# Attention and two feed-forward layers on one core: a second layer put into the next slot, rest tiles' products taken in turn, and a one-row product put last

## The chip, the core and the metric
The kernel runs on one core of one Trainium2 chip. A core has TensorE (matrix products, PE in the profile; its weight loads are shown apart as PEld), VectorE (DVE), ScalarE (ACT), GpSimd (POOL) and SyncE (SP, which here only issues transfers). The engines run side by side and wait for each other through semaphores. The metric is the device time of one execution in microseconds (us), lower is better. Before the change the median of three runs is 1379.33 us (1378.09 to 1381.95).

## The reference
Three stages follow one another, for 4 batches of 576 tokens, 8 heads of 64 and a model width of 512:

```
scores = q @ k.T / 8
kth    = the 32nd largest of each row of scores
attn   = softmax of the scores that are >= kth, 0 elsewhere
x      = attn @ v                                   # heads joined to (4, 576, 512)

u  = x + real(fft over tokens of fft over width of x)
un = (u - mean) / sqrt(var + 1e-6)
y  = u + relu(un @ w_ch1) @ w_ch2                   # 512 -> 2048 -> 512

xn  = (y - mean) / sqrt(var + 1e-6) * g_ln
out = y + relu(xn @ w_ch1') @ w_ch2'                # own weights
```

## The kernel before
The program is written by hand, engine by engine. Each engine walks through numbered slots s; what stands in a slot is fixed in the code, and semaphores make an engine wait where another one is late. One attention tile of up to 128 score rows by 576 belongs to each of the slots 0 to 143 (36 for a batch); after slot 143 only feed-forward work and the last batch's transform are left.

*The attention tile.* VectorE finds the 32 largest of a row in four rounds (MAX8 and MATCH_REPLACE8, function `pair`, two tiles at a time) and then multiplies the exponentials by the mask (L1122). ScalarE makes the exponentials (`exps`, L902), copies scores out of PSUM (`scores_out`, L868) and, for the second half of the tiles, reads scores that were made early and put aside in memory (`scores_in`, L891, a transfer). TensorE turns a masked tile in five transposes (`probs_T`, L667), ScalarE copies the result (`probs_out`, L909), and TensorE multiplies it by v (`values`). For two heads of 64 columns each these products write 64 PSUM partitions each, taken in turn (L690). The last 64 rows of 576 make a rest tile: its two heads stand in one tile, rows 0 to 63 and 64 to 127. There are four rest tiles in a batch, in the slots 8, 9, 26 and 27 of its 36, 16 in all. Their products are at L684: first all five chunks of one head, then all five of the other, the last chunk with 64 rows instead of 128.

*The feed-forward layers.* The work is cut into 224 units (`NUNITS`): one unit is a group of two or three token chunks by 128 of the 2048 hidden columns. `mlp1(n)` (L719) is the unit's first layer, 12 products; ScalarE's `relu_out(n)` (L962, L963) writes the hidden values, GpSimd's `unit(n)` (L500) their low part; `mlp2(n)` (L736) is the second layer, 6 or 9 products. Most slots hold one unit: in slot s TensorE does `mlp1` of that slot's unit and, after `values(s)`, `mlp2` of the last unit of slot s - 1 (`closing_at`). Twelve slots (`DOUBLE`: 52, 66, 86, 90, 96, 101, 105, 111, 121, 126, 132, 138) hold two units, n - 1 and n. The second one comes at the slot's end, after `values_back`: `mlp1(n)`, then `mlp2(n - 1)`. On ScalarE `relu_out(n)` and `highs(n)` (rounding the next units' weights, L977, L982) stand at the slot's end too.

*The transform.* The Fourier transforms are products with cosine and sine tables. A batch has ten pieces (`dft_piece(b, i)`): four over tokens, six over width (i = 4 to 9, `wid`, L775). The pieces 4, 6 and 8 add a product with one row (`alt`, L779) in the midst of an accumulation. For batches 1 and 2 a piece is made in two halves (`sides`), two pieces in each of the slots 78 to 82 and 116 to 120; batch 0's are done together in slot 37 (`SEAM`), batch 3's after the attention.

VectorE can be at most four tiles ahead of TensorE (`RING`), and TensorE can't turn a tile before VectorE has masked it. SyncE issues the weights' transfers in order; each waits for the product that last used its buffer (L444, L455, L460).

Of the kernel before, what the change touches and what calls it, by code (L numbers as in the profile page):

```python
# [8 lines left out]
P = 128  # L9
CF = S // P  # L10
TAIL = S - CF * P
C = CF + 1
# [67 lines left out]
def units_at(s):  # L80

    return [n for n in range(NUNITS) if slot_of(n) == s]
# [20 lines left out]
def second_at(s):  # L103

    return units_at(s)[1:] if s in DOUBLE else []
# [30 lines left out]
def width(c):  # L136

    return P if c < CF else TAIL
# [69 lines left out]
def build(nc, q, k, v, g2, w_raw, seq_t, wid_t, alt_t, w_low, sc_ahead, out):  # L208
# [4 lines left out]
    with ctx:  # L213
        def sb(name, shape, dt=f32):
            return ctx.enter_context(nc.sbuf_tensor(name, shape, dt))
# [13 lines left out]
        alt = sb("alt", [1, EO])  # L229
        gb = sb("gb", [P, DM])  # L230
        vn = sb("vn", [P, 2, C, 2, D + 1])
# [8 lines left out]
        pT = sb("pT", [P, 2, C * P])  # L240
# [7 lines left out]
        aT = sb("aT", [P, 4, SO])  # L248
# [23 lines left out]
        PV = Tp[:, C * P:C * P + D + 1]  # L272
# [332 lines left out]
        def _(pe):  # L605
            def scores(s):
                b, i = divmod(s, NT)
                hp, c, head = tile_of(i)
                par = hp % 2
                if i == first_tile(hp):  # L610
                    pe.wait_ge(s_qk[par], 2 * 16 * ((NHP // 2) * b + hp // 2 + 1))
                if s >= 2:
                    pe.wait_ge(s_sc_sb, s - 1 if s < RING else s)
                if c == CF:
                    for half in range(2):
                        n = slice(half * HALF, (half + 1) * HALF)
                        for h in range(2):
                            o, hd = slice(h * TAIL, (h + 1) * TAIL), slice(h * D, (h + 1) * D)
                            last = nc.tensor.matmul(Sp[o, half, 0:HALF], qT[hd, par, CF * P:S], kT[hd, par, n],
                                                    start=True, stop=True)  # L620
                else:
                    n = slice(head * HALF, (head + 1) * HALF)
                    for h in range(2):
                        hd = slice(h * D, (h + 1) * D)
                        last = nc.tensor.matmul(score_banks(s)[:, h, 0:HALF], qT[hd, par, c * P:(c + 1) * P], kT[hd, par, n],  # L625
                                                start=True, stop=True)
                last.then_inc(s_sc_ps, 1)
# [42 lines left out]
            def values(s):  # L670
                b, i = divmod(s, NT)
                hp, t, head = tile_of(i)
                par = hp % 2
                if head == 0:
                    return
                if i <= first_tile(hp) + 1:
                    pe.wait_ge(s_v[par], 3 * 16 * ((NHP // 2) * b + hp // 2 + 1))
                pe.wait_ge(s_pT_sb, s + 1)
                if t == CF:
                    for h in range(2):  # L680
                        o = slice(h * TAIL, (h + 1) * TAIL)
                        for c in range(C):
                            w = width(c)
                            last = nc.tensor.matmul(PV[o, :], pT[0:w, i % 2, c * P + o.start:c * P + o.stop],  # L684
                                                    vn[0:w, par, c, h, :], start=(c == 0), stop=(c == C - 1))
                    last.then_inc(s_pv_ps, 1)
                    return
                for c in range(C):
                    for h in range(2):
                        last = nc.tensor.matmul(OT[h * D:(h + 1) * D, :], vn[:, par, c, h, 0:D], pT[:, h, c * P:(c + 1) * P],  # L690
                                                start=(c == 0), stop=(c == C - 1))
                last.then_inc(s_pv_ps, 2)
# [50 lines left out]
            def dft_piece(b, i):  # L743
                if i == 0:
                    pe.wait_ge(s_fold, b + 1)
                    if b in (1, 2):
                        pe.wait_ge(s_rem, b)
                if b == 0:
                    if i == 0:
                        pe.wait_ge(s_ah_sb, AHEAD)  # L750
                    if i >= 4:
                        pe.wait_ge(s_pc_sb, max(4, i - 3))
                else:
                    pe.wait_ge(s_pc_sb, PIECES * b + i)
                    if b < B - 1:
                        pe.wait_ge(s_sc_sb, min(piece_slot(b, i) + RING + 1, KEPT))
                where, (sides, n) = piece(b, i), piece_cols(b, i)
                for side in range(sides):
                    o, col = where[:, side, :], slice(side * n, (side + 1) * n)
                    if i < 4:  # L760
                        for kc in range(J):
                            r = slice(0, P) if kc < HP else rest(b)
                            last = nc.tensor.matmul(o, xf[r, kc, i // 2, (i % 2) * P:(i % 2 + 1) * P], seq[r, i // 2, kc, col],  # L763
                                                    start=(kc == 0), stop=(kc == J - 1))
                            if i == 2 and kc == 0:

                                for km in range(J):
                                    r = slice(0, P) if km < HP else rest(b)
                                    mid = xs[:, 0, km, FOLD:FOLD + 1] if km < HP else U[r, chunk(b, CF), FOLD:FOLD + 1]
                                    nc.tensor.matmul(o[0:1, :], mid, seq[r, 0, km, col], start=False, stop=False)  # L770
                    else:
                        j, part = divmod(i - 4, 2)
                        to = slice(j * P, j * P + (P if j < HP else TAIL))
                        for kk in range(2):
                            last = nc.tensor.matmul(o, aT[:, 2 * part + kk, to], wid[:, part, kk, col],  # L775
                                                    start=(kk == 0), stop=(kk == 1))
                            if part == 0 and kk == 0:

                                nc.tensor.matmul(o, aT[0:1, 2, to], alt[0:1, col], start=False, stop=False)  # L779
                last.then_inc(s_pc_ps, 1)  # L780

            def un_T(t):
# [26 lines left out]
            for s in range(SLOTS):  # L809
                pieces = [(b, i) for b in range(B) for i in range(PIECES) if piece_slot(b, i) == s]  # L810
                units = units_at(s)
                if s < TILES:
                    if turns_at(s - 1):
                        pe.wait_ge(s_unT_sb, last_turn(s))
                    probs_T(s)
                    if s + RING < KEPT and s not in SCORED.values():
                        if last_piece(s) > last_piece(s - 1) > 0 or last_piece(s) == PIECES and s == SEAM + 1:
                            pe.wait_ge(s_pc_sb, last_piece(s))
                        scores(s + RING)
                if s == START[0]:  # L820
                    for t in turns_at(s):
                        un_T(t)
                if s != START[0]:
                    for n in units:
                        if n not in second_at(s):
                            mlp1(n)
                    for t in turns_at(s):
                        un_T(t)
                if s != SEAM and pieces:
                    dft_piece(*pieces[0])  # L830
                if s < TILES:
                    values(s)
                for n in closing_at(s):
                    mlp2(n)
                if s != SEAM and pieces:
                    dft_piece(*pieces[1])
                if s < TILES:
                    values_back(s)
                for n in second_at(s):
                    mlp1(n)  # L840
                    mlp2(n - 1)
                if 0 < s <= AHEAD:
                    scores_ahead(s - 1)
                if s == SEAM:
                    pe.wait_ge(s_tab, 48)
                    for b, i in pieces:
                        dft_piece(b, i)
                if s == START[0]:
                    for n in units:
                        mlp1(n)  # L850
                        if n > 0:
                            mlp2(n - 1)
                        if n in SCORED:
                            scores(SCORED[n] + RING)
# [504 lines left out]
```

## Time and profile before
| | |
|---|---|
| median of 3 runs | 1379.33 us |
| the profiled execution | 1380.66 us, of which span 1378.9 us |
| TensorE busy | 1271.3 us, 92% of the span |
| VectorE busy | 1113.0 us, 81% |
| ScalarE busy | 789.3 us, 57% |
| GpSimd busy | 348.8 us, 25% |
| granted TensorE clock, mean | 0.971 of full speed |

The span runs from the first to the last instruction; the profiled execution's own time is 1.8 us more. A busy TensorE is not one at its peak: its products are pipelined, so a row's duration is longer than the step from one start to the next, and what a group costs is read from its start to the start of what follows. Times in the rows are counted from the span's start.

### The profile page before, as it was taken

The numbers are of one execution on the slowest core, as the hardware profiler recorded it, in microseconds if no ns is written. First come the engines' busy times: TensorE is split into PE (matmuls) and PEld (weight loads), VectorE is DVE, ScalarE is ACT, GpSimd is POOL, SyncE is SP. The second block draws the span as 40 slices with busy tenths as digits, with TensorE's granted clock in tenths as the row PEclk, the third lists the DMA queues.
The fourth block names the chain that finished last, engine by engine and source line by source line (L and its number), as shares of the span: only waits on it lengthen the run. The fifth ranks groups of instructions, "written<-read, shape, count | busy, mean of one in ns | idle before, by whom it ended". The sixth has DMA issues, their size and how long they took to land.

```text
span 1378.9 us, 22760 instructions
## 1 busy us (share of the span) xinstructions
PE 1271.3 (92%) x7944; PEld 1037.2 (75%) x7944; DVE 1113.0 (81%) x2224; ACT 789.3 (57%) x1564; POOL 348.8 (25%) x308
## 2 busy tenths in 40 slices
PE   5877778999999699799998999999999999999999
PEld 2444444777777578688887788888689999999998
DVE  7999999999999988999889789975485555555553
ACT  4777765677777456575665556654344434444442
POOL 3444430122122341132233222322121121212110
PEclk8998989999999999999999999999999999999999
DMA  7899993566757656787786467663244343333342
GB/s 258 310 339 340 328 340 129 186 218 207 245 180 257 191 187 216 247 272 237 231 281 225 155 230 243 218 229 131 76 165 143 121 156 120 130 123 123 122 146 84
DMA packets 117396, 280.63 MB, mean 204 GB/s; under 512 B 29730, under 2 KB 29731, under 8 KB 117283
## 3 DMA queue, kind: packets, MB, share of 16 engines
q1 hardware_dynamic: 105522, 231.98, 51.0%
q10 hardware_dynamic: 10368, 42.47, 8.1%
q0 software_dynamic: 1392, 4.73, 1.0%
q8 instruction: 65, 1.06, 0.3%
q14 instruction: 49, 0.39, 0.1%
HBM read 235.87 MB, written 42.73 MB: 202 GB/s over the span
## 4 chain that ended last, share of the span: by engine, by line
PE 62%; DVE 30%; issue 4%; POOL 1%; ACT 1%; DMA 1%; SPq 0%; DVEq 0%; ACTq 0%; POOLq 0%
PE Big L736 24%; PE Big L719 17%; DVE top L1109 13%; DVE wk L1115 12%; PE Sp L719 7%; PE Tp L667 3%; DVE ex L1122 3%; PE Tp L690 2%; PE Sp L763 2%; PE Tp L684 1%; PE Sp L775 1%; DVE st L1201 1%; PE Tp L794 1%; PE Sp L625 1%; PE Big L763 1%
## 5 line engine op out<-in xcount | busy, mean ns | idle before, releaser
L736 PE MATMUL Big<-wr,hh 128*128 128x512 f32 x1152 | 362.6, 396 | 0.0
L719 PE MATMUL Big<-uh,wr 128*128 128x256 f32 (+1 forms) x1384 | 317.2, 319 | 7.4 <-ACT hh L963 7.4
L1109 DVE MAX8 top<-wk 128x8 f32<-128x576 f32 x432 | 304.4, 746 | 0.0
L719 PEld LDWEIGHTS Big<-uh,wr 128*128 128x128 f32 x1384 | 233.0, 191 | 26.8 <-issue 18.7
L736 PEld LDWEIGHTS Big<-wr,hh 128*128 128x128 f32 x1152 | 217.9, 189 | 41.7
L736 PE MATMUL Big<-wr,hl 128*128 128x512 f32 x576 | 238.3, 414 | 3.6 <-DVE wr L1254 2.6
L500 POOL TENSOR_TENSOR hl<-hf,hh 128x256 fp32r<-128x256 f32 (+1 forms) x123 | 105.3, 856 | 471.7 <-ACT hh L963 471.6
L719 PE MATMUL Big<-ul,wr 128*128 128x256 f32 (+1 forms) x692 | 215.5, 311 | 0.0
L1115 DVE MATCH_REPLACE8 wk<-top,wk 128x576 f32<-128x576 f32 x288 | 211.5, 741 | 0.0
L667 PE MATMUL Tp<-ident,ex 128*128 128x128 f32 x720 | 120.8, 295 | 50.5 <-DVE ex L1122 46.7
L909 ACT ACTIVATE pT<-Tp 128x640 f32<-128x640 f32 x144 | 101.4, 704 | 112.3 <-PE Tp L667 112.0
L667 PEld LDWEIGHTS Tp<-ident,ex 128*128 128x128 f32 x720 | 89.7, 150 | 94.1 <-issue 60.7
L963 ACT ACTIVATE hh<-Big 128x256 fp32r<-128x256 f32 (+1 forms) x173 | 74.6, 431 | 119.1 <-PE Big L719 119.1
L1122 DVE SCALAR_TENSOR_TENSOR ex<-sc,top,ex 128x576 f32<-128x576 f32 x144 | 119.7, 869 | 25.6 <-ACT ex L902 25.6
L719 PEld LDWEIGHTS Big<-ul,wr 128*128 128x128 f32 x692 | 132.5, 192 | 0.0
L736 PEld LDWEIGHTS Big<-wr,hl 128*128 128x128 f32 x576 | 108.8, 189 | 31.1 <-issue 10.8
L1109 DVE MAX8 top<-sc 128x8 f32<-128x576 f32 x144 | 101.6, 747 | 20.5 <-DMA sc<-sc_ahead 13.5
L1115 DVE MATCH_REPLACE8 wk<-top,sc 128x576 f32<-128x576 f32 x144 | 105.7, 741 | 0.0
L902 ACT ACTIVATE ex<-sc,nmx 128x576 f32<-128x576 f32 x144 | 103.9, 769 | 2.3
L494 POOL TENSOR_TENSOR wr<-wf,wr 128x1024 fp32r<-128x1024 f32 x32 | 75.3, 2369 | 111.3 <-DVE top L1109 110.6
L719 PE MATMUL Sp<-uh,wr 128*128 128x384 f32 (+1 forms) x408 | 99.9, 329 | 0.0
L962 ACT ACTIVATE hf<-Big 128x256 f32<-128x256 f32 (+1 forms) x123 | 50.8, 413 | 74.2 <-PE Big L719 74.2
(133 smaller groups left out, 1859.3 us busy)
## 6 DMA issues: line engine op xcount, KB each, us to landing
wf<-in_weights SPq DMA_DIRECT2D x206, 512.0 KB, 3.6
wr<-w_low SPq DMA_DIRECT2D x246, 256.0 KB, 4.3
sc<-in_weights SPq DMA_DIRECT2D x50, 512.0 KB, 3.3
sc<-sc_ahead ACTq DMA_DIRECT2D x36, 576.0 KB, 5.5
w_low<-wr SPq DMA_DIRECT2D x32, 512.0 KB, 6.5
sc_ahead<-U ACTq DMA_DIRECT2D x18, 576.0 KB, 4.7
sc_ahead<-un ACTq DMA_DIRECT2D x9, 576.0 KB, 4.0
sc_ahead<-yb ACTq DMA_DIRECT2D x9, 576.0 KB, 6.3
```

The costliest lines, as they stand in the source:

```text
L494: pool.tensor_tensor(wr[:, r, :, 1, :], wf[:, j % WFS, :, :], wr[:, r, :, 0, :].bitcast(f32), ALU.subtract).then_inc(s_wlow, 1)
L500: pool.tensor_tensor(hl[:, n % 2, 0:w], hf[:, n % 2, 0:w], hh[:, n % 2, 0:w].bitcast(f32), ALU.subtract).then_inc(s_hl[0], 1)
L667: last = nc.tensor.transpose(Tp[:, c * P:(c + 1) * P], ex[:, s % RING, c * P:(c + 1) * P], ident[:, :])
L719: last = nc.tensor.matmul(hidden(n), a[:, kd * P:(kd + 1) * P], x[:, kd, 0:P * SIZE[p]], start=(kd == 0 and j == 0), stop=(kd == KD - 1 an ...
L736: last = nc.tensor.matmul(Ac[:, j, :], a[:, n % 2, j * P:(j + 1) * P], w, start=(f == 0 and m == 0), stop=(f == KF - 1 and m == 2))
L902: nc.scalar.activation(ex[:, s % RING, 0:S], sc[:, s % RING, :], ACT.Exp, bias=nmx[:, s % RING:s % RING + 1], scale=1.0 / np.sqrt(D)).then ...
L909: nc.scalar.activation(pT[:, s % 2, :], Tp[:, 0:C * P], ACT.Copy).then_inc(s_pT_sb, 1)
L962: nc.scalar.activation(hf[:, n % 2, 0:w], hidden(n), ACT.Relu)
L963: nc.scalar.activation(hh[:, n % 2, 0:w], hidden(n), ACT.Relu).then_inc(s_h_sb, 1)
L1109: nc.vector.max(top[:, s % RING, r, :], src).then_inc(s_top, 1)
L1115: nc.vector.match_replace(out=wk[:, a, :], in_to_replace=top[:, s % RING, r, :], in_values=src, imm_value=STRUCK).then_inc(s_struck, 1)
L1122: nc.vector.scalar_tensor_tensor(out=ex[:, s % RING, 0:S], in0=sc[:, s % RING, :], scalar=top[:, s % RING, ROUNDS - 1, 7:8], in1=ex[:, s % ...
```

## The change
Three edits, all on TensorE.

1. The second layer of a double slot's first unit, `mlp2(n - 1)`, moves from the end of slot s, behind `mlp1(n)`, to slot s + 1: behind that slot's transposes and scores, in front of its `mlp1`.
2. The rest tile's products go chunk by chunk with the two heads in turn, all of them over 128 rows (the added rows of the last chunk are zeros on one side).
3. In the width pieces of the transform the one-row product comes after all products of the piece, for both halves together, and ends the accumulation.

```diff
@@ values(s), rest tile
-                    for h in range(2):
-                        o = slice(h * TAIL, (h + 1) * TAIL)
-                        for c in range(C):
-                            w = width(c)
-                            last = nc.tensor.matmul(PV[o, :], pT[0:w, i % 2, c * P + o.start:c * P + o.stop],
-                                                    vn[0:w, par, c, h, :], start=(c == 0), stop=(c == C - 1))
+                    for c in range(C):
+                        for h in range(2):
+                            o = slice(h * TAIL, (h + 1) * TAIL)
+                            last = nc.tensor.matmul(PV[o, :], pT[:, i % 2, c * P + o.start:c * P + o.stop],
+                                                    vn[:, par, c, h, :], start=(c == 0), stop=(c == C - 1))
@@ dft_piece(b, i), i >= 4
                             last = nc.tensor.matmul(o, aT[:, 2 * part + kk, to], wid[:, part, kk, col],
-                                                    start=(kk == 0), stop=(kk == 1))
-                            if part == 0 and kk == 0:
-
-                                nc.tensor.matmul(o, aT[0:1, 2, to], alt[0:1, col], start=False, stop=False)
+                                                    start=(kk == 0), stop=(kk == 1 and part == 1))
+                if i >= 4 and (i - 4) % 2 == 0:
+                    for side in range(sides):
+                        col = slice(side * n, (side + 1) * n)
+                        last = nc.tensor.matmul(where[:, side, :], aT[0:1, 2, to], alt[0:1, col], start=False, stop=True)
@@ the loop over slots, after probs_T(s) and scores(s + RING)
+                for n in second_at(s - 1):
+                    mlp2(n - 1)
@@ at the slot's end
                 for n in second_at(s):
                     mlp1(n)
-                    mlp2(n - 1)
```

TensorE's order before, from the end of slot 105's `mlp1(n)` into slot 106 (L719 is `mlp1`, L736 `mlp2`, L667 the transposes of slot 106):

```order
L719 MATMUL Big<-uh,wr 128x384 x2
L719 MATMUL Big<-ul,wr 128x384
L736 MATMUL Big<-wr,hl 128x512
L736 MATMUL Big<-wr,hh 128x512 x2
L736 MATMUL Big<-wr,hl 128x512
L736 MATMUL Big<-wr,hh 128x512 x2
L736 MATMUL Big<-wr,hl 128x512
L736 MATMUL Big<-wr,hh 128x512 x2
L667 MATMUL Tp<-ident,ex 128x128 x5
L719 MATMUL Big<-uh,wr 128x256 x2
```

The same place now (L718 is `mlp1`, L735 `mlp2`):

```order
L718 MATMUL Big<-uh,wr 128x384 x2
L718 MATMUL Big<-ul,wr 128x384
L667 MATMUL Tp<-ident,ex 128x128 x5
L735 MATMUL Big<-wr,hl 128x512
L735 MATMUL Big<-wr,hh 128x512 x2
L735 MATMUL Big<-wr,hl 128x512
L735 MATMUL Big<-wr,hh 128x512 x2
L735 MATMUL Big<-wr,hl 128x512
L735 MATMUL Big<-wr,hh 128x512 x2
L718 MATMUL Big<-uh,wr 128x256 x2
```

The nine products of the second layer have changed places with the five transposes; nothing else moved, and the rows of the other four engines are in the same order as before.

TensorE before, in slot 80, from a width piece of the transform (L775, L779) to the rest tile (L684) and the closing second layer:

```order
L775 MATMUL Sp<-wid,aT 128x129
L779 MATMUL Sp<-alt,aT 128x129
L775 MATMUL Sp<-wid,aT 128x129 x2
L779 MATMUL Sp<-alt,aT 128x129
L775 MATMUL Sp<-wid,aT 128x129
L684 MATMUL Tp<-vn,pT 64x65 x10
L736 MATMUL Big<-wr,hl 128x512
```

The same place now:

```order
L774 MATMUL Sp<-wid,aT 128x129 x4
L779 MATMUL Sp<-alt,aT 128x129 x2
L683 MATMUL Tp<-vn,pT 64x65 x10
L735 MATMUL Big<-wr,hl 128x512
```

The products are as many as before; the one-row products now stand behind one another. The ten of the rest tile stand in one row in both, since the rows don't tell the heads apart.

## Rows read from the trace of the kernel before

**Rows 1.** The page: busy tenths in 40 slices, and the chain's shares by engine

```profile
DVE  7999999999999988999889789975485555555553
...
PE 62%; DVE 30%; issue 4%; POOL 1%; ACT 1%; DMA 1%; SPq 0%; DVEq 0%; ACTq 0%; POOLq 0%
```

**Rows 2.** Busy time by stretch: us, each engine busy (count), clock, DMA

```profile
0.00:218.00 218.00, 156.51 (x1084) 95.42 (x1084) 210.92 (x451) 151.13 (x237) 79.26 (x44) 0.90 0.87 308
...
825.00:1379.00 554.00, 546.56 (x2961) 480.51 (x2959) 339.34 (x581) 254.07 (x501) 108.26 (x92) 1.00 0.44 146
```

**Rows 3.** Timeline, VectorE: start us, us, operation [idle before <-releaser]

```profile
347.29 1.42 DVE L1109 MAX8 top<-sc 128x8 f32<-128x576 f32 x2 [0.48 <-ACT sc L868]
...
534.81 0.82 DVE L1122 SCALAR_TENSOR_TENSOR ex<-sc,top,ex 128x576 f32<-128x576 f32 x1 [4.62 <-ACT ex L902]
...
695.60 1.42 DVE L1109 MAX8 top<-sc 128x8 f32<-128x576 f32 x2 [3.22 <-DMA sc<-sc_ahead]
...
808.27 0.82 DVE L1122 SCALAR_TENSOR_TENSOR ex<-sc,top,ex 128x576 f32<-128x576 f32 x1 [6.02 <-ACT ex L902]
```

**Rows 4.** Timeline, TensorE, the transposes of slots 90 and 126

```profile
581.42 1.30 PE L667 MATMUL Tp<-ident,ex 128*128 128x128 f32 x5 [5.41 <-DVE ex L1122]
...
824.73 0.74 PE L667 MATMUL Tp<-ident,ex 128*128 128x128 f32 x5 [1.17 <-DVE ex L1122]
```

**Rows 5.** Timeline, weight loads of slot 98's rest tile, first of each stretch

```profile
635.26 0.13 PEld L684 LDWEIGHTS Tp<-vn,pT 128*64 128x64 f32 x1 [0.25 <-issue]
...
635.87 0.13 PEld L684 LDWEIGHTS Tp<-vn,pT 64*64 64x64 f32 x1
...
636.13 0.13 PEld L684 LDWEIGHTS Tp<-vn,pT 128*64 128x64 f32 x1
...
636.74 0.13 PEld L684 LDWEIGHTS Tp<-vn,pT 64*64 64x64 f32 x1
...
636.99 0.19 PEld L736 LDWEIGHTS Big<-wr,hl 128*128 128x128 f32 x1
```

**Rows 6.** Timeline, a tile of whole rows in slot 97: products, first four loads

```profile
628.76 1.31 PE L690 MATMUL Tp<-pT,vn 128*64 128x128 f32 x20
...
628.76 0.20 PEld L690 LDWEIGHTS Tp<-pT,vn 128*64 128x64 f32 x4 [0.25 <-issue]
```

**Rows 7.** Timeline, TensorE, width piece of slot 81 and what follows

```profile
526.10 0.38 PE L775 MATMUL Sp<-wid,aT 128*128 128x129 f32 x2
526.41 0.48 PE L779 MATMUL Sp<-alt,aT 1*128 1x129 f32 x2
526.83 0.71 PE L775 MATMUL Sp<-wid,aT 128*128 128x129 f32 x4
527.47 0.48 PE L779 MATMUL Sp<-alt,aT 1*128 1x129 f32 x2
527.89 0.49 PE L775 MATMUL Sp<-wid,aT 128*128 128x129 f32 x2
528.30 0.27 PE L684 MATMUL Tp<-vn,pT 128*64 128x65 f32 x1
```

**Rows 8.** Timeline, TensorE and ScalarE, from slot 105 into slot 106

```profile
686.33 0.39 PE L736 MATMUL Big<-wr,hl 128*128 128x512 f32 x1
...
688.42 0.71 PE L667 MATMUL Tp<-ident,ex 128*128 128x128 f32 x5
...
689.17 0.71 ACT L909 ACTIVATE pT<-Tp 128x640 f32<-128x640 f32 x1 [0.73 <-PE Tp L667]
689.18 0.33 ACTq L891 DMA_DIRECT2D sc<-sc_ahead  x1
```

**Rows 9.** Timeline, VectorE and TensorE, slot 111 into slot 112

```profile
718.56 0.99 DVE L1122 SCALAR_TENSOR_TENSOR ex<-sc,top,ex 128x576 f32<-128x576 f32 x1
...
720.06 0.40 PE L736 MATMUL Big<-wr,hl 128*128 128x512 f32 x1
...
721.45 0.71 PE L667 MATMUL Tp<-ident,ex 128*128 128x128 f32 x5
```

## The prediction, as it was put on record before the change was run

> **What bounds the kernel now.** I read the page first. Its busy digits show VectorE at nine tenths or more in nearly all of the first 17 slices and falling later, and its chain has 62% on TensorE and 30% on VectorE [rows 1]. So there is no single bound; the two take turns. The busy times by stretch then show the ends of the picture: to 218 us VectorE works 210.9 of 218 us, so nothing that TensorE saves there can count, and from 825 us on TensorE works 546.6 of 554 us at the full clock, so everything counts [rows 2]. Between them I looked for the places where one engine hands the bound to the other, which are the waits of VectorE and of TensorE's transposes. VectorE waits at 347.29 for scores that ScalarE copies out (0.48 us), at 534.81 for slot 82's exponentials (4.62), at 695.60 for a transfer of early scores (3.22) and at 808.27 for exponentials (6.02) [rows 3]; each of these was issued behind a `probs_out` that waited for TensorE, so up to there TensorE set the pace. In the other direction the transposes wait for VectorE's mask at 581.42 (slot 90, 5.41 us) and at 824.73 (slot 126, 1.17) [rows 4].
>
> That gives this alternation: VectorE up to about 482 us (with one link to TensorE at 347); TensorE to 534.8; VectorE to 581.4; TensorE from slot 90 through slot 106 (688.4) and over the transfer to 695.6; VectorE to slot 116 (about 746); TensorE to 808.3; VectorE to 824.7; TensorE to the end. A saving on TensorE counts only inside its own stretches. It is passed on at a handover as long as the engine that receives it had waited for longer, which the waits of 4.62, 3.22 and 6.02 us allow.
>
> **Edit 2, the rest tile.** Before, the 20 records (two for each of ten products) took from 635.26 to 636.99, 1.73 us [rows 5]. The row starts split that into stretches: 8 records with 128 rows 0.61 us, 2 with 64 rows 0.26, 8 again 0.61, 2 again 0.25. The shape changes between the stretches vanish (three of them), since all products now have 128 rows and 64 columns. That alone gives one stretch of 20 at one record a time: 0.25 + 18 x 0.06 = 1.33 us, 0.40 saved.
>
> The tile of whole rows has the same two-heads-in-turn order. Its 20 records, with 128 moving columns instead of 65, take 1.31 us by the row's duration, while one after another at 0.06 x 128/65 = 0.118 each they would take 2.4 [rows 6]. So products on the two column halves do run side by side. Its first four weight loads are done within 0.20 us though a single one takes 0.13 [rows 5, 6], so the loads overlap as well. With both overlapping, the rest tile costs 0.25 + 8 x 0.06 + 0.02, about 0.75 us, and saves 1.0. The bounds are 0.40 and 1.1; I take 1.0, since rows 6 are the same instruction form but for the moving columns.
>
> The Trainium skill (TensorEngine Tiling (Array Packing), Key Properties) says that changing the tiling mode drains the engine and that different tiles load and multiply in parallel; rows 5 and 7 show the drain as some 0.14 to 0.2 us a change. It also has a rule against this edit: TensorE: Matmul & The Clock Gate, Part 3, has weight loads overlap running products only when the row group differs. Here both heads use all rows, so by it nothing would be gained beyond the changes of shape (the second rival); rows 6 speak against it.
>
> Of the 16 rest tiles those of slots 8, 9, 26, 27 lie under VectorE's work before 218 us, and 62, 63 in its stretch up to 482: nothing. 44 and 45 make the scores for 347.29 come about 2 us earlier, but VectorE waits only 0.48 there, so they give 0.48. In TensorE's stretches lie 80, 81 (before 534.8), 98, 99 (before 688.4), 116, 117 (before 808.3) and 134, 135 (at the end): eight tiles, 8.0 us.
>
> **Edit 3, the one-row product.** In slot 81 the piece has five stretches: 0.31, 0.42, 0.64, 0.42 and 0.41 us [rows 7]. Two more records in a stretch cost 0.64 - 0.41 = 0.23. Now there are eight `wid` records (0.31 + 3 x 0.23 = 1.00) and four one-row ones (0.42 + 0.23 = 0.65): 1.65 against 2.20, 0.55 saved, since two of four changes of shape are gone. That holds where the next product has another shape anyway (a rest tile or `values` behind it: slots 80, 81, 119). In 118 and 120 the second layer follows, which now pays for the refill, some 0.1 (0.41 - 0.31 of rows 7), and starts less early: 0.35 each. In slot 82 it lies behind the handover. Sum 3 x 0.55 + 2 x 0.35 = 2.35 us. With one side (batches 0 and 3) two changes stay two; only the refill moves to the next product: 0, bounds -0.1 and +0.1 for each of six.
>
> **Edit 1, the moved second layer.** TensorE's work is the same, so in a stretch that TensorE bounds it is worth nothing by itself. What it changes is that slot s + 1's transposes come one `mlp2` earlier, 2.09 us for a group of three chunks (686.33 to 688.42) and 1.39 for two (720.06 to 721.45) [rows 8, 9]. ScalarE can't use all of it: in front of `probs_out` it still has `relu_out(n)` and `highs(n)`. At slot 106 its idle time before `probs_out` is 0.73 us [rows 8], and that is the gain of the copy, of the exponentials behind it and of the transfer issued at 689.18. This transfer releases VectorE at 695.60, a handover, so 0.73 us count. Ends: 0 if the transfer's 6.4 us grow by as much; 2.1 if it also lands sooner because it now goes ahead of the weight transfer that `mlp2` releases. I take 0.73. At slot 53 the gain falls under the same 0.48 as above. At the ten other double slots no handover hangs on `probs_out(s + 1)`: 0.
>
> The price could be a new wait: behind the transposes now queue `mlp2(n - 1)`, `mlp1(n + 1)` and all that follows. The tightest place that I found is slot 112: its mask ends at 718.56 + 0.99 = 719.55, and the transposes would start at 720.06, when the second layer starts now [rows 9]. So 0.5 us are left there, and it lies in a stretch that VectorE bounds until 746: nothing. Ahead of `mlp1(n + 1)` stand the same products as before, so the wait for `relu_out(n)` has the same cover. SyncE's transfer for the buffer that `mlp2(n - 1)` frees goes out later by the five transposes, 0.5 to 0.7 us, for a unit three further on: hidden.
>
> **The sum.** 0.48 + 8.0 + 2.35 + 0.73 = 11.6 us. The profiled execution would go from 1380.66 to 1369.1; it lies 1.33 us above the median, and I take the difference from the median: 1379.33 - 11.6 = 1367.7 us.
>
> **The clock.** After the wait of 5.41 us the five transposes of slot 90 take 1.30 us, against 0.71 elsewhere [rows 4, 9]: the lower level of 1.2 GHz instead of 2.4. Slot 90 starts a TensorE stretch, so how long the lower level lasts there counts. The change shifts that moment by some us; I allow 2 us either way.
>
> **The rivals.**
> *Side by side in products only.* The weight loads go one after another; the tile costs 1.33 us, eight tiles give 3.2, the sum is 6.8 and the time 1372.5. For it: 64-column loads follow at 0.06 us in rows 5, and twice that also fits the pace of rows 6. Against it: four loads in 0.20 us. 15%.
> *The gains don't pass the handovers.* The stretches end on something that I read as TensorE's but that VectorE or the transfers set; then only the two tiles after 825 us and part of the rest count, 2 to 4 us, about 1376.5. Against it: the waits of VectorE are long. 10%.
> *A new wait in front of the transposes.* Because TensorE gets faster and reaches the transposes 1.4 to 2.1 us earlier, VectorE's mask comes too late in the double slots, and `mlp2(n - 1)`, which used to fill that time, is queued behind. It decides from the point where the mask ends after the start of the moved `mlp2`; slot 112 is 0.5 us short of it [rows 9]. The price is up to 2.1 us a slot, and clock on top: with all twelve it would be some 20 us against a gain of 11.6, so about 1386, and slower than before needs at least six of them in TensorE's own stretches. 4%.
> *The forecast.* 66%, its own range 1365.0 to 1370.5. The remaining 5% are a larger gain (the transfer sooner, a shorter time at the low clock): about 1363.
>
> **Range and chances.** From the larger gains to the side-by-side rival and its spread: 1363.5 to 1374.0. A measurement here tells about 0.3%, 4.1 us, from no change. Faster by more than that holds the forecast, the first rival, the larger gain and a little of the second: 0.87. Within it: 0.09. Slower: 0.04.
>
> **What would show it.** The rest tile's 20 records at about 0.75 us to the next start, with no 64-row form left; 1.33 means the first rival. The two-sided `alt` records as four in a row in a piece of about 1.65 us. In slots 53, 67, 87 and so on the transposes before the second layer. VectorE's wait at 347 gone, `probs_out(106)` without an idle time before it. Slot 90 starting some 3.6 us earlier, slot 116 some 6.3, slot 126 some 9.6. The prediction is wrong if TensorE's waits for the mask grow in TensorE's own stretches, or if these slots start earlier by much less than that.

## The result, and the profile after

The changed kernel takes 1363.94 us (median of four, 1362.52 to 1364.60), the kernel before 1380.64 us beside it: a ratio of 0.9879, 95% interval 0.9867 to 0.9892, or 16.7 us less. Forecast were 11.6 us less. The profiled executions are 1364.6 and 1380.66 us, their spans 1362.8 and 1378.9, 16.1 us apart. The rows below are held against these two spans, slot by slot. A slot starts where its transposes (L667) start.

From the page after, the lines that answer to [rows 1]:

```profile
DVE  7999999899999997999899889976585454646453
...
PE 57%; DVE 35%; issue 5%; POOL 1%; ACT 1%; DMA 1%; SPq 0%; DVEq 0%; ACTq 0%; POOLq 0%
```

The picture is the same, with a little of the chain gone from TensorE to VectorE. The timeline after, VectorE, at the four places of [rows 3] (start us, us, operation, [idle before <- releaser]):

```profile
345.19 0.77 DVE L1110 MAX8 top<-sc 128x8 f32<-128x576 f32 x1
...
529.27 0.82 DVE L1123 SCALAR_TENSOR_TENSOR ex<-sc,top,ex 128x576 f32<-128x576 f32 x1 [1.50 <-ACT ex L903]
...
684.12 0.76 DVE L1110 MAX8 top<-sc 128x8 f32<-128x576 f32 x1
...
794.27 0.82 DVE L1123 SCALAR_TENSOR_TENSOR ex<-sc,top,ex 128x576 f32<-128x576 f32 x1 [5.58 <-ACT ex L903]
```

The waits of 0.48 and 3.22 us are gone, the one of 4.62 is down to 1.50. The transposes of slots 90 and 126, as in [rows 4], with slot 116 between them:

```profile
575.91 0.44 PE L667 MATMUL Tp<-ident,ex 128*128 128x128 f32 x1 [5.42 <-DVE ex L1123]
...
735.92 0.30 PE L667 MATMUL Tp<-ident,ex 128*128 128x128 f32 x1 [2.17 <-DVE ex L1123]
...
810.73 0.30 PE L667 MATMUL Tp<-ident,ex 128*128 128x128 f32 x1 [1.17 <-DVE ex L1123]
```

Slot 90 starts 5.5 us earlier (581.42 before), slot 116 10.6 (746.54), slot 126 14.0 (824.73). Forecast were 3.6, 6.3 and 9.6.

The rest tile of slot 98 and the width piece of slot 81 after, answering to [rows 5] and [rows 7]:

```profile
629.57 0.80 PE L683 MATMUL Tp<-vn,pT 128*64 128x65 f32 x20
630.30 0.50 PE L735 MATMUL Big<-wr,hl 128*128 128x512 f32 x1
...
522.14 1.05 PE L774 MATMUL Sp<-wid,aT 128*128 128x129 f32 x8
523.13 0.71 PE L779 MATMUL Sp<-alt,aT 1*128 1x129 f32 x4
523.76 0.28 PE L683 MATMUL Tp<-vn,pT 128*64 128x65 f32 x2
```

The tile takes 0.73 us to the next start (forecast 0.75, before 1.73), the piece 1.62 us (forecast 1.65, before 2.20). So what each product costs was read rightly; what was missed lies in how it reaches the end.

Where the 16.1 us come from, by how much earlier slots start than before:

| from slot to slot | gained, us | forecast | what |
|---|---|---|---|
| 0 to 78 | 2.3 | 0.5 | rest tiles 44, 45, and collisions on VectorE |
| 78 to 90 | 3.2 | 3.1 | rest tiles 80, 81, two pieces |
| 90 to 106 (the transposes' own step of 2.1 us left out) | 2.2 | 2.0 | rest tiles 98, 99 |
| 106 to 116 | 2.9 | 0.7 | the transfer of slot 106 |
| 116 to 126 | 3.4 | 3.25 | rest tiles 116, 117, three pieces |
| 126 to the end | 2.1 | 2.0 | rest tiles 134, 135 |

Two of six rows are wrong, and they hold 4.0 of the 4.5 us that were missed. The clock has little part in this table: the mean granted clock is 0.87 in both profiles from slot 76 to 78, 0.82 and 0.84 from slot 90 to 92 (14.31 and 14.11 us), and 1.00 in both in slot 116. The transition from slot 105 to 106 after, TensorE and then ScalarE, answering to [rows 8]:

```profile
678.65 0.71 PE L667 MATMUL Tp<-ident,ex 128*128 128x128 f32 x5
679.12 0.48 PE L735 MATMUL Big<-wr,hl 128*128 128x512 f32 x1
```

```profile
678.85 0.49 ACT L963 ACTIVATE hf<-Big 128x384 f32<-128x384 f32 x1 [1.77 <-PE Big L718]
679.24 0.49 ACT L964 ACTIVATE hh<-Big 128x384 fp32r<-128x384 f32 x1
679.41 0.33 ACTq L892 DMA_DIRECT2D sc<-sc_ahead  x1
679.61 0.63 ACT L983 ACTIVATE wr<-wf 128x512 fp32r<-128x512 f32 x1
680.13 0.64 ACT L978 ACTIVATE wr<-wf 128x512 fp32r<-128x512 f32 x1
680.65 0.70 ACT L910 ACTIVATE pT<-Tp 128x640 f32<-128x640 f32 x1
```

ScalarE's idle time before the copy (L910) is gone, as forecast. But the transfer (ACTq) stands at 679.41, in the midst of ScalarE's work and before the copy that precedes it in the program. It went out 9.77 us earlier than the 689.18 of [rows 8], while slot 105 started only 7.68 us earlier: the whole second layer of 2.09 us, not 0.73.

### The profile page after: what moved, and what is told of

Read it like the earlier page. It is cut to its first block, busy times and chain, and to the rows that moved or that the text cites. A ratio compares the mean times of both kernels' runs of the same rounds, so it can differ in the third digit from the quotient of the medians.

```text
span 1362.8 us, 22760 instructions
## 1 busy us (share of the span) xinstructions
PE 1245.7 (91%) x7944; PEld 1019.1 (75%) x7944; DVE 1112.6 (82%) x2224; ACT 786.3 (58%) x1564; POOL 350.7 (26%) x308
## 4 chain that ended last, share of the span: by engine, by line
PE 57%; DVE 35%; issue 5%; POOL 1%; ACT 1%; DMA 1%; SPq 0%; DVEq 0%; ACTq 0%; POOLq 0%
PE Big L735 23%; PE Big L718 15%; DVE top L1110 15%; DVE wk L1116 14%; PE Sp L718 7%; DVE ex L1123 3%; PE Tp L667 3%; PE Tp L689 2%; PE Sp L762 2%; PE Sp L774 1%; DVE st L1202 1%; PE Tp L794 1%; PE Big L762 1%; DMA sc<-sc_ahead 0%; PE Big L774 0%
## 5 line engine op out<-in xcount | busy, mean ns | idle before, releaser
L735 PE MATMUL Big<-wr,hh 128*128 128x512 f32 x1152 | 361.9, 395 | 0.0
L718 PE MATMUL Big<-uh,wr 128*128 128x256 f32 (+1 forms) x1384 | 315.5, 318 | 6.2 <-ACT hh L964 5.7
L718 PEld LDWEIGHTS Big<-uh,wr 128*128 128x128 f32 x1384 | 233.3, 191 | 26.2 <-issue 16.2
L735 PEld LDWEIGHTS Big<-wr,hh 128*128 128x128 f32 x1152 | 217.7, 189 | 41.3
L735 PE MATMUL Big<-wr,hl 128*128 128x512 f32 x576 | 239.1, 415 | 3.6 <-DVE wr L1255 2.6
L718 PE MATMUL Big<-ul,wr 128*128 128x256 f32 (+1 forms) x692 | 215.3, 311 | 0.0
L667 PE MATMUL Tp<-ident,ex 128*128 128x128 f32 x720 | 117.3, 289 | 55.7 <-DVE ex L1123 50.5
L910 ACT ACTIVATE pT<-Tp 128x640 f32<-128x640 f32 x144 | 101.1, 702 | 108.0 <-PE Tp L667 107.8
L667 PEld LDWEIGHTS Tp<-ident,ex 128*128 128x128 f32 x720 | 86.5, 146 | 96.1 <-issue 63.3
L735 PEld LDWEIGHTS Big<-wr,hl 128*128 128x128 f32 x576 | 109.0, 189 | 32.4 <-issue 12.1
L718 PEld LDWEIGHTS Big<-ul,wr 128*128 128x128 f32 x692 | 132.2, 191 | 0.0
L718 PE MATMUL Sp<-uh,wr 128*128 128x384 f32 (+1 forms) x408 | 100.0, 329 | 0.0
L689 PE MATMUL Tp<-pT,vn 128*64 128x128 f32 x1280 | 86.5, 283 | 11.6 <-ACT pT L910 11.3
```

The costliest lines, as they stand in the source:

```text
L667: last = nc.tensor.transpose(Tp[:, c * P:(c + 1) * P], ex[:, s % RING, c * P:(c + 1) * P], ident[:, :])
L718: last = nc.tensor.matmul(hidden(n), a[:, kd * P:(kd + 1) * P], x[:, kd, 0:P * SIZE[p]], start=(kd == 0 and j == 0), stop=(kd == KD - 1 an ...
L735: last = nc.tensor.matmul(Ac[:, j, :], a[:, n % 2, j * P:(j + 1) * P], w, start=(f == 0 and m == 0), stop=(f == KF - 1 and m == 2))
L910: nc.scalar.activation(pT[:, s % 2, :], Tp[:, 0:C * P], ACT.Copy).then_inc(s_pT_sb, 1)
```

## The experiments

Twelve kernels were run. "Against before" is the ratio to the kernel before, measured beside it; the changed kernel stands at 0.9879 (0.9867 to 0.9892). The changed kernel was not measured beside them, so what a run is said to differ from it is the difference of two ratios, each known to 1.2 to 2.3 us either way.

**Each edit by itself.** The kernel before with only the moved second layer (edit 1):

```diff
+                for n in second_at(s - 1):
+                    mlp2(n - 1)
...
                 for n in second_at(s):
                     mlp1(n)
-                    mlp2(n - 1)
```

> The kernel before with edit 1 alone (the moved second layer). Theory A (the transfer of early scores is issued by ScalarE's queue and not by ScalarE itself, so at slot 106 it moves by the whole second layer, 2.09 us, and also lands sooner): VectorE's waits of 0.62 and 3.22 us at 690.81 and 695.60 are gone, time 3 to 4 us shorter. Rival B (as the prediction had it, ScalarE's idle time of 0.73 us is all there is to win): 0.7 to 1.2 us shorter, VectorE's wait of 3.22 us shrinks to about 2.5.

Against before 0.9972 (0.9961 to 0.9984), 3.8 us less. The transfer and VectorE's next two steps in that run:

```profile
686.21 0.33 ACTq L892 DMA_DIRECT2D sc<-sc_ahead  x1
```

```profile
689.47 0.81 DVE L1123 SCALAR_TENSOR_TENSOR ex<-sc,top,ex 128x576 f32<-128x576 f32 x1
690.20 0.09 DVE L1123 DVE_READ_ACCUMULATOR ex<-sc,top,ex 128x1 f32 x1
690.20 0.82 DVE L1123 SCALAR_TENSOR_TENSOR ex<-sc,top,ex 128x576 f32<-128x576 f32 x1
690.94 0.09 DVE L1123 DVE_READ_ACCUMULATOR ex<-sc,top,ex 128x1 f32 x1
690.94 1.42 DVE L1110 MAX8 top<-sc 128x8 f32<-128x576 f32 x2
```

There is no wait left where 0.62 and 3.22 us were. Theory A holds, B falls. In its profile 2.95 us are gained between slot 105 and slot 116; the other 0.9 us are 1.55 gained in slots 76 and 77, where the granted clock differs and no double slot lies (the last section shows it), less 0.6 lost around slot 38.

Only the rest tiles (edit 2), the diff being that of the change:

```diff
-                    for h in range(2):
...
-                        for c in range(C):
...
+                    for c in range(C):
+                        for h in range(2):
...
```

> The kernel before with edit 2 alone (rest tiles). Both theories: the rest tile takes 0.73 us to the next start, eight tiles in TensorE's own stretches give 8.0 us and the two before 347 us give 0.5. Theory A adds that VectorE's mask operation at 311.36 loses its collision with GpSimd (1.82 us back to 0.82) because TensorE comes 2 us earlier there, so 9.5 to 10.5 us in all. Rival B: 8.5 us.

Against before 0.9926 (0.9912 to 0.9939), 10.2 us less. That is theory A's range. In its profile slot 72 starts 2.35 us earlier, as in the changed kernel (2.33), so what comes before 482 us beyond the 0.48 belongs to this edit and its moment.

Only the one-row product last (edit 3):

```diff
-                            if part == 0 and kk == 0:
...
-                                nc.tensor.matmul(o, aT[0:1, 2, to], alt[0:1, col], start=False, stop=False)
+                if i >= 4 and (i - 4) % 2 == 0:
+                    for side in range(sides):
...
```

> The kernel before with edit 3 alone (the one-row product last). From the trace after: a two-sided piece 1.62 us instead of 2.20 or 2.03, a one-sided one 1.59 instead of 1.51. Slots 80, 81, 118, 119, 120 count: 0.58 + 0.58 + 0.41 + 0.58 + 0.43 = 2.6, less 3 x 0.085 for batch 3: 2.3 us shorter. A rival that the refill behind the piece costs as much as it gives: 0.

Against before 0.9980 (0.9970 to 0.9989), 2.8 us less (1.5 to 4.1), where the forecast's own sum was 2.35. The refill rival falls. Where the pieces stand, this run's profile gains 1.1 us from slot 78 to 90 and 1.4 from 118 to 121, 2.5 in all. The three add up: 3.8 + 10.2 + 2.8 = 16.8 us, against 16.7 for all together. That they meet so closely is luck, since each is known only to 1.3 to 1.9 us either way.

**Where edit 1 works.** The second layer moved at slot 105 alone:

```diff
-                for n in second_at(s - 1):
+                for n in second_at(s - 1) if (s - 1) == 105 else []:
                     mlp2(n - 1)
...
                     mlp1(n)
+                    if not (s == 105):
+                        mlp2(n - 1)
```

> The kernel before with the second layer moved at slot 105 alone. Theory A: this one slot carries edit 1's worth, so within 0.5 us of the run with all twelve moved, 3 to 4 us shorter than before. Rival C (the other eleven slots give something too, by the exponentials of slots 91 and 102): clearly less than that run.

Against before 0.9977 (0.9969 to 0.9986), 3.2 us less. One slot of twelve carries nearly all; the difference of 0.6 us to all twelve lies inside both intervals. The profiles tell more: both runs gain the same 2.95 us between slot 105 and slot 116, and the run with all twelve gains nothing further between 78 and 105 or behind 116. No gain of the other eleven slots is seen.

**The transfer's moment.** The changed kernel with one wait added, so that ScalarE's queue holds the transfer back until the copy of slot 106 is done:

```diff
             def scores_in(n):
...
+                if 2 * n - RING == 106:
+                    act.wait_ge(s_pT_sb, 107)
```

> The changed kernel, but ScalarE's queue issues slot 106's transfer of early scores only when the copy of slot 106 is done (one added wait). Theory A (it is the early issue that edit 1 brings at slot 106): issued about 1.9 us later, landing after 684.1, so VectorE waits 2 to 3 us for it again, and the time is 2 to 3 us longer than the changed kernel. Rival B (the transfer was issued when ScalarE was free anyway, or its moment doesn't matter): no change.

Against before 0.9898 (0.9885 to 0.9912), 1366.37 us, some 2.5 us more than the changed kernel, though the two intervals overlap a little. ScalarE and VectorE in that run:

```profile
679.52 0.70 ACT L912 ACTIVATE pT<-Tp 128x640 f32<-128x640 f32 x1
680.25 0.36 ACTq L894 DMA_DIRECT2D sc<-sc_ahead  x1
```

```profile
687.04 0.76 DVE L1112 MAX8 top<-sc 128x8 f32<-128x576 f32 x1 [3.77 <-DMA sc<-sc_ahead]
```

Now the queue waits for the copy, and VectorE's wait is back. The profile is plainer than the times: from slot 105 to slot 116 this run gains nothing on the kernel before (8.81 us ahead, then 8.77), where the changed kernel gains 2.9. Everything else of edit 1 is still in place, so it is this transfer that gives the gain.

**The rest tile taken apart.** The changed kernel with one head after the other, all over 128 rows:

```diff
-                    for c in range(C):
-                        for h in range(2):
+                    for h in range(2):
+                        for c in range(C):
```

> The changed kernel, but with the rest tile's ten products one head after the other (all over 128 rows). It parts the shape from the order. Theory A (loads and products of the two column halves run side by side): without the turns the tile takes 1.31 to 1.33 us instead of 0.73, eight tiles, 4.7 us longer than the changed kernel. Rival (only the changes of shape counted): 0.73 us stay and the time is the same.

Against before 0.9907 (0.9894 to 0.9921), 1367.69 us, 3.8 us more than the changed kernel (4.7 expected). In slot 98:

```profile
629.69 1.20 PE L683 MATMUL Tp<-vn,pT 128*64 128x65 f32 x20
630.83 0.50 PE L735 MATMUL Big<-wr,hl 128*128 128x512 f32 x1
```

1.14 us, between the 1.33 that the prediction worked out for a strict line and the 0.73 in turn. So the order is worth 0.4 us a tile and the shape 0.6. The forecast had them 0.6 and 0.4: even with the heads one after the other, the second head's first products start while the first head's last ones are under way. The single records show it: seven of them start between 630.09 and 630.27, where one head alone has a start every 0.06 us.

The heads in turn, but the last chunk with 64 rows:

```diff
                     for c in range(C):
+                        w = width(c)
...
-                            ... pT[:, i % 2, ...], vn[:, par, c, h, :]
+                            ... pT[0:w, i % 2, ...], vn[0:w, par, c, h, :]
```

> The changed kernel, but the last chunk again with 64 rows; the heads stay in turn. One change of shape stands inside the tile. Theory A: 0.73 + 0.14 to 0.17 = about 0.88 us a tile, some 1.2 us longer than the changed kernel. Rival (a change of shape costs nothing once products run side by side): 0.73 us and the same time.

Against before 0.9884 (0.9870 to 0.9897), 1364.68 us. In slot 98:

```profile
628.84 0.95 PE L684 MATMUL Tp<-vn,pT 128*64 128x65 f32 x20
629.72 0.50 PE L736 MATMUL Big<-wr,hl 128*128 128x512 f32 x1
```

0.88 us: one change of shape costs 0.15 us, as read from [rows 5]. On the whole time the 1.2 us expected are 0.7, inside what these times can tell.

**The collision.** What made up the 1.8 us more before slot 78? Held against each other, VectorE's rows shift in jumps at its mask operations (L1122). GpSimd and VectorE in the kernel before, and then in the changed one:

```profile
310.69 1.87 POOL L507 TENSOR_TENSOR ul<-uf,uh 128x512 fp32r<-128x512 f32 x1 [0.23 <-ACT uf L953]
...
311.36 1.82 DVE L1122 SCALAR_TENSOR_TENSOR ex<-sc,top,ex 128x576 f32<-128x576 f32 x1
```

```profile
308.71 1.28 POOL L507 TENSOR_TENSOR ul<-uf,uh 128x512 fp32r<-128x512 f32 x1 [0.23 <-ACT uf L954]
...
311.10 0.82 DVE L1123 SCALAR_TENSOR_TENSOR ex<-sc,top,ex 128x576 f32<-128x576 f32 x1
```

The same operations take 1.82 and 1.87 us here and 0.82 and 1.28 where they don't overlap. The mask operation just before it (310.63, 0.80 us) was beside GpSimd's too and was not slowed: it came first, and then it was GpSimd's that got longer. A kernel before in which GpSimd waits for the masks at slot 46:

```diff
                 pool.wait_ge(s_unT_sb, t + 1)
+                if turn_slot(t) == 46:
+                    pool.wait_ge(s_masked, 50)
                 pool.tensor_tensor(ul...
```

> The kernel before, but at slot 46 GpSimd starts its subtraction (L507) only when VectorE's mask operations 48 and 49 are done. Theory A (the mask operation of 1.82 us at 311.36 is held up by the GpSimd operation beside it, 1.0 us lost, in a stretch that VectorE bounds): that operation takes 0.8 us, all later slots up to 482 us start 1.0 us earlier and the time is 1.0 us shorter, less if another collision takes its place. Rival (the 1.82 us have another reason, such as the copies on ScalarE): the operation stays at 1.8 us.

Against before 1.0001 (0.9992 to 1.0011): no change. GpSimd, then VectorE there:

```profile
311.77 1.30 POOL L509 TENSOR_TENSOR ul<-uf,uh 128x512 fp32r<-128x512 f32 x1 [1.86 <-DVE ex L1124]
```

```profile
310.81 0.81 DVE L1124 SCALAR_TENSOR_TENSOR ex<-sc,top,ex 128x576 f32<-128x576 f32 x1
311.55 0.08 DVE L1124 DVE_READ_ACCUMULATOR ex<-sc,top,ex 128x1 f32 x1
312.30 0.76 DVE L1111 MAX8 top<-sc 128x8 f32<-128x576 f32 x1 [0.67 <-ACT sc L870]
```

The mechanism is shown: without GpSimd beside it the mask takes 0.81 us. A gain in time, expected at 1.0 us, is not: VectorE now waits 0.67 us for scores that ScalarE copies out, which come from TensorE. In the changed kernel TensorE is 2 us earlier there, so that wait does not appear. By these rows the collision was worth something only together with the rest tiles of slots 44 and 45; no run has those tiles' gain without the end of the collision, so this is argued. The Trainium skill (SBUF — State Buffer, Who interferes with whom) has this as a rule, a port pair that VectorE's operations with two SBUF inputs and GpSimd's lock against each other; these rows agree.

**Versions that follow from this.** If the moment at which an input reaches VectorE is what counts, it can be moved by itself. In the changed kernel, ScalarE makes the exponentials of slots 84 and 85 one slot earlier (EARLY_EXPS = (82,)); or the transfers and exponentials of slots 104 and 106 go one slot earlier (both tuples (104, 106)):

```diff
...
                     x_back(s)
+                if s + 1 in EARLY_IN:
+                    scores_in((s + 1 + RING) // 2)
+                if s + 1 in EARLY_EXPS:
+                    exps(s + 3)
+                    exps(s + 4)
...
```

> The changed kernel, with the exponentials of tiles 84 and 85 made by ScalarE at the end of slot 81 instead of behind slot 82's copy. If what counts at a handover is when the next input reaches VectorE (theory A), VectorE's wait of 1.50 us at 529.27 shrinks to about 0.5 and all to slot 90 comes 1.0 us earlier: 1.0 us shorter than the changed kernel. Rival: TensorE's later copy takes it back, no change.

> The changed kernel, with the transfers of slots 104 and 106 issued, and their exponentials made, at the end of slots 103 and 105. Theory A: VectorE's wait of 3.51 us at 673.00 is mostly gone and slot 116 starts 2 to 3 us earlier, 2 to 3 us shorter than the changed kernel, less what a collision with GpSimd or the low clock takes. Rival: TensorE bounds this stretch already (its waits of 0.8, 3.4 and 2.2 us before slot 116 are needed for something else): no change.

Against before 0.9883 (0.9866 to 0.9899) and 0.9879 (0.9865 to 0.9894), both the same as the changed kernel. In the second VectorE's wait of 3.51 us at 673.00 shrank, but did not go, and a new one stands behind it. The changed kernel, then this run:

```profile
673.00 0.76 DVE L1110 MAX8 top<-sc 128x8 f32<-128x576 f32 x1 [3.51 <-DMA sc<-sc_ahead]
```

```profile
671.24 0.76 DVE L1119 MAX8 top<-sc 128x8 f32<-128x576 f32 x1 [2.53 <-DMA sc<-sc_ahead]
...
683.06 0.76 DVE L1119 MAX8 top<-sc 128x8 f32<-128x576 f32 x1 [0.61 <-DMA sc<-sc_ahead]
```

From slot 104 to 116 that profile gains 0.8 us on the changed kernel's, not 2 to 3. I took the transfer for the only thing in the way, and the next transfer was close behind. In the first, VectorE's wait of 1.50 us went, and 1.13 us of waiting came up in slot 91.

The exponentials of tiles 124 and 125 in slot 122 instead of 123:

```diff
-    return s // 2 in (NT + 7, NT + 8, NT + 9, 3 * NT // 2 + 7, 3 * NT // 2 + 8, 3 * NT // 2 + 9)
+    return s // 2 in (NT + 7, NT + 8, NT + 9, 3 * NT // 2 + 8, 3 * NT // 2 + 9)
```

> The changed kernel, with the exponentials of tiles 124 and 125 made in slot 122 instead of 123. VectorE's wait of 5.58 us at 794.27 ends some 5 us earlier, so TensorE's wait of 1.17 us at slot 126 is gone and it bounds the kernel from slot 116 to the end: 1.2 us shorter than the changed kernel. Rival: the hidden values of slot 122's unit come 1.5 us later from ScalarE and TensorE waits for them: no change or slower.

Against before 0.9868 (0.9853 to 0.9882), 1361.93 us: 1.5 us less than the changed kernel by the ratios, with intervals that overlap. In the profile slot 126 has no wait any more, and gains 1.3 us on slot 124, as expected.

> The changed kernel with all three of the moves above. Theory A: the handovers are independent, so the sum of the three, 4 to 5 us shorter than the changed kernel, about 1359.5 us. Rival: less than the largest of them.

Against before 0.9867 (0.9852 to 0.9882), 1361.74 us. That is the third one's gain and nothing of the others; the expected sum of 4 to 5 us fell with them. The two kernels with this edit are the two lowest medians of all.

## Why the prediction was right, and where it was short

The direction, the mechanism of the largest term and its size were right, and the time lay in the range, near its lower end. It lay outside the forecast's own range of 1365.0 to 1370.5, though, in the "larger gain" that had 5%. Of the 4.5 us missed, profile against profile, 2.2 are one transfer and 1.8 come before slot 78, most of them by chance.

*What bounds.* The alternation held: after the change the transposes wait at the same slots, and the handovers pass the gains on. The rival in which they don't falls with the table.

*Rest tiles, 8.0 us.* Right: 1.00 us a tile, eight tiles. The split into shape (0.4) and order (0.6) was the wrong way round. The rival with loads in a line (the first in its list, though the text calls it the second) falls.

*One-row product, 2.35 us.* Right, 2.8 us measured alone. A two-sided piece gained 0.58 with a rest tile behind it and 0.41 to 0.43 before a second layer, where I had 0.55 and 0.35. The prediction counted two of four changes of shape as gone. With a product of yet another shape behind the piece, three of five are, and 0.58 us for three and 0.42 for two make about 0.2 each. Of the three one-sided pieces at the end two cost 0.09 and one gained 0.14.

*Before 482 us, 0.48 us.* The step that failed first. The wait of 0.48 was gone, but I had taken VectorE's rows between the waits as fixed. Some mask operations there were 0.2 to 1.0 us longer than the others, in the trace before already. With TensorE 1 to 2 us earlier three of them (at 311.36, 345.01 and 405.58: 1.82, 1.05 and 1.16 us) no longer collided, and one at 382.00 did a little more (1.13, then 1.30). At 369.46 the delay only passed from one mask operation to the next and gave nothing. That makes some 1.4 us; a second wait for scores, 0.17 us at 300.97, went too. The collisions' part is chance: it comes from where things fall, not from what the edit does.

*Edit 1, 0.73 us.* The step that failed most: "ScalarE can't use all of it", and so "the gain of the copy, of the exponentials behind it and of the transfer issued at 689.18". For the transfer it is wrong: it is issued by the queue, once TensorE's transposes are done, while ScalarE still works off what is ahead. So it moved by 2.09 us, and it landed in 4.5 us instead of 6.4. It now goes out ahead of the weight transfers (the next at 680.27) and not behind them (687.95, 688.62 and 688.98); that this is why it landed sooner is likely, and not shown by itself. VectorE's waits of 0.62 and 3.22 us vanished; a later collision and a slower operation gave 0.9 us back, and 2.9 us are left. The upper end of this term was 2.1 us, for the case that the transfer also lands sooner. That was the right case, but even its figure was too low: what counts is the length of VectorE's waits, not how far the copy or the transfer moves.

*No new wait in the double slots.* Nearly right. At slot 112, called 0.5 us short of it, the transposes now wait 0.56 us for the mask, because VectorE had gained less than TensorE there (10.6 against 11.5 us); as forecast it lies in VectorE's stretch and costs nothing.

*A sum.* The price of that rival, 20 us against a gain of 11.6, would give about 1388 us and not 1386; nothing else rests on it.

*The clock.* Slot 90 took its 1.2 GHz time as before. In the runs of single edits it did move elsewhere, as the last section shows.

## What to carry to other kernels

Where two engines take turns as the bound, find each handover and ask what exactly is handed over. A saving counts up to the next handover and is capped by the wait there, and a queue may issue a transfer before its engine has done what stands ahead of it, so an edit that only changes an order can be worth as much as the wait was long. Look also at operations of one kind that take longer than their fellows: those can be collisions that any shift in time undoes or brings about, and a forecast needs a range for them.

## What the runs showed of the hardware

**ScalarE's queue runs ahead of ScalarE.** In the changed kernel the transfer behind the copy in program order is issued at 679.41, and the copy itself starts at 680.65.

**Products on the two column halves overlap even in a line of one head and then the other.** 20 records take 1.14 us; at the pace of [rows 5] a strict line would take 1.33, an estimate.

**Half clock at the wrong place costs 1.5 us.** Slot 116 begins a stretch that TensorE bounds. Busy time in that slot, in the kernel before and in the run where GpSimd waits for the masks (columns as in [rows 2]):

```profile
746.54:756.39 9.85, 9.85 (x68) 7.94 (x68) 9.85 (x21) 4.59 (x10) 1.96 (x2) 1.00 0.58 199
```

```profile
745.55:756.94 11.39, 11.39 (x67) 9.31 (x68) 11.39 (x24) 4.60 (x10) 1.96 (x2) 0.85 0.44 143
```

TensorE's work is the same (68 weight loads in both), the granted clock is 1.00 and 0.85, and the slot takes 1.54 us more. In both TensorE had waited for the mask just before (1.27 and 2.17 us). The changed kernel's profile had the longer wait too and full clock behind it, so the wait alone does not settle it. The same step appears around slot 77. Slots 76 and 77 in the kernel before, and then with edit 1 alone, which moves nothing there:

```profile
482.36:495.35 12.99, 10.72 (x73) 8.99 (x72) 12.99 (x26) 7.87 (x17) 11.03 (x10) 0.87 0.65 208
```

```profile
483.82:494.44 10.62, 9.17 (x74) 7.72 (x72) 10.62 (x23) 7.75 (x17) 9.44 (x10) 1.00 0.69 242
```

TensorE is busy 1.55 us less for the same work, at a clock of 1.00 instead of 0.87. Single times of the same kernel differ by up to 5 us (1374.78 to 1379.73 with edit 3 alone). Two spans, each from one profile, therefore do not tell a change of 1.5 us. The small terms above rest on the repeated times, or on stretches of slots in which the clock is the same.
